# Own buffers for the first loads, the first weight's split on three engines, and the order of exponentials and copies on ScalarE

## What is computed

```python
scores = scale * q @ k.T
bias = -(cum[:, None] - cum[None, :])          # cum = cumsum(max(s, 0))
scores = where(causal, -1e9, scores + minimum(bias, 0))
attn = exp(scores - max); attn = attn / (sum + 1e-9)
x = attn @ v                                   # heads side by side: 2304 x 512
# first network (512 -> 1024 -> 512)
h = x @ w_in; solu = h * softmax(h); ln = (solu - mean) / sqrt(var + 1e-6) * g_ln
x2 = ln @ w_out
# second network (512 -> 2048 -> 512)
h = x2 @ w2_in; out = (h * clip(h + 3, 0, 6) / 6) @ w2_out
```

## Time and profile before

| what | value |
|---|---|
| median of 3 runs | 928.36 us (926.16 to 928.52) |
| profiled execution | 927.4 us, span 925.6 us |
| TensorE busy | 846.5 us (91%) |
| VectorE, ScalarE, GpSimd busy | 437.2, 407.7, 307.9 us |
| attention with the first network | up to about 449 us for the attention items |
| first hidden matmul | at 64.98 us |

### The profile page before, as it was taken

The page is one execution under the profiler, slowest core; times in us unless marked ns, Lnnn a source line. Parts: engine busy times, 40 slices in busy tenths (PEclk is TensorE's granted clock), DMA queues, the critical chain, the costliest instruction groups (busy, mean ns, idle before and its releaser), DMA issues.

```text
span 925.6 us, 13793 instructions
## 1 busy us (share of the span) xinstructions
PE 846.5 (91%) x4912; PEld 753.1 (81%) x4912; DVE 437.2 (47%) x1057; ACT 407.7 (44%) x901; POOL 307.9 (33%) x419
## 2 busy tenths in 40 slices
PE   5676878999899998999898999999999999999997
PEld 4555767878788887788787899999989898989996
DVE  3536677666676767766645232222232322232222
ACT  5636576656755566566323244322232322232222
POOL 5894375545654456545156244000000000000000
PEclk9879879999999999999999999999999999999999
DMA  6736333434333234322212040000000000000000
GB/s 180 222 101 206 99 104 120 136 94 116 119 119 95 85 117 131 108 93 72 72 65 93 1 137 1 35 1 1 34 1 1 35 1 1 35 1 1 35 1 34
DMA packets 39139, 67.11 MB, mean 73 GB/s; under 512 B 4448, under 2 KB 16736, under 8 KB 39072
## 3 DMA queue, kind: packets, MB, share of 16 engines
q1 hardware_dynamic: 39072, 66.23, 23.1%
HBM read 61.42 MB, written 4.79 MB: 72 GB/s over the span
## 4 chain that ended last, share of the span: by engine, by line
PE 71%; DVE 9%; ACT 8%; POOL 6%; issue 5%; DMA 1%; SPq 0%; DVEq 0%; ACTq 0%; POOLq 0%
PE psum L742 10%; PE psum L791 7%; PE psum L793 7%; PE psum L809 7%; PE psum L792 7%; PE psum L810 7%; PE psum L808 7%; PE psum L712 4%; PE psum L687 3%; PE psum L771 3%; DVE es L953 2%; PE psum L673 2%; ACT prob L1065 2%; ACT p_hi L1088 2%; PE psum L668 2%
## 5 line engine op out<-in xcount | busy, mean ns | idle before, releaser
L1019 DVE SCALAR_TENSOR_TENSOR act<-act,psum 128x384 f32<-128x384 f32 x96 | 53.2, 554 | 287.2 <-ACT act L1160 287.2
L1160 ACT ACTIVATE act<-psum,three 128x384 f32<-128x384 f32 x96 | 55.7, 580 | 285.8 <-PE psum L793 285.8
L791 PE MATMUL psum<-x_hi,w_hi 128*128 128x384 f32 x384 | 129.5, 337 | 0.9 <-DVE x_lo L979 0.9
L793 PE MATMUL psum<-x_hi,w_lo 128*128 128x384 f32 x384 | 129.5, 337 | 0.0
L792 PE MATMUL psum<-x_lo,w_hi 128*128 128x384 f32 x384 | 129.0, 336 | 0.0
L810 PE MATMUL psum<-w_hi,g_lo 128*128 128x512 f32 x288 | 113.9, 395 | 0.0
L809 PE MATMUL psum<-w_lo,g_hi 128*128 128x512 f32 x288 | 113.7, 395 | 0.0
L893 DVE TENSOR_TENSOR p_lo<-psum,p_hi 128x512 fp32r<-128x512 f32 (+2 forms) x128 | 71.9, 572 | 86.9 <-ACT p_hi L1088 86.4
L808 PE MATMUL psum<-w_hi,g_hi 128*128 128x512 f32 x288 | 112.0, 389 | 0.0
L1088 ACT ACTIVATE p_hi<-psum 128x512 fp32r<-128x512 f32 (+2 forms) x128 | 62.2, 499 | 111.3 <-PE psum L687 79.8
L771 PE MATMUL psum<-lnT_hi,w_out_hi 128*128 128x256 f32 x288 | 83.3, 289 | 12.4 <-DVE xT L975 12.4
(11 more groups left out here) (91 smaller groups left out, 1891.1 us busy)
## 6 DMA issues: line engine op xcount, KB each, us to landing
qk_raw<-qk SPq DMA_DIRECT2D x32, 480.0 KB, 3.5
qk_raw<-qk SPq DMA_DIRECT2D x32, 256.0 KB, 2.7
bias<-cum_dram SPq DMA_DIRECT2D x32, 256.0 KB, 3.9
v_raw<-v_rows SPq DMA_DIRECT2D x32, 160.0 KB, 2.7
bias_tail<-cum_dram SPq DMA_DIRECT2D x32, 144.0 KB, 3.2
out<-out_sb SPq DMA_DIRECT2D x6, 768.0 KB, 3.5
bias<-cum_dram SPq DMA_DIRECT2D x32, 128.0 KB, 3.4
w_raw<-w_in SPq DMA_DIRECT2D x16, 256.0 KB, 3.2
```

Source lines behind the costliest of these rows:

```text
L791: pe.matmul(ps, w2_hi[f][:, cols], xh, start=(c_ == 0), stop=False)
L793: last = pe.matmul(ps, w2_lo[f][:, cols], xh, start=False, stop=(c_ == NC - 1))
```

## The change

There are five parts. The eight loads of the first batch's first-kind units get buffers of their own, in the region that `w_out` takes later, so that they and the next three are issued without a wait, and the splits of queries and keys are placed one item earlier in general. The bias of the first unit comes from two TensorE matmuls (a column of the identity, broadcast, times `cum`) and two ScalarE copies in place of DMAs. `w_in` is loaded and split in 8 pieces: ScalarE makes all high parts, VectorE the first 4 low parts, GpSimd the other 4, and each hidden matmul of the first tile waits for its own piece. In ScalarE's loop the exponentials of item n+1 stand in front of `copy_probs(n)`. And `STARTS` moves tiles 0 to 9 up to two items earlier and ends one item earlier.

```diff
-STARTS = [14, 23] + [32 + 7 * i for i in range(4)] + [60 + 6 * i for i in range(8)] + [109, 116, 122, 128, 134]
+STARTS = [12, 21, 31, 37, 44, 51, 59, 65, 71, 77, 84, 90, 96, 102, 109, 115, 121, 127, 133]
...
-W_IN_PARTS = 16
+
+W_IN_PARTS = 8
+W_IN_DVE = 4
...
+OWN = HEADS
...
+def buffer_of(load):
+
+    return 3 + load if load < OWN else (load - OWN) % 3
...
-    SPLIT_AT.setdefault(BASE[_u] - (3 if _u % (2 * PAIRS) <= PAIRS else 4), []).append((_u, 0))
-    SPLIT_AT.setdefault(BASE[_u] - 2, []).append((_u, 1))
+    for _e in range(2):
+        if load_of(_u, _e) < OWN:
+            _n = max(-3, load_of(_u, _e) - 5)
+        elif _u == PAIRS:
+            _n = BASE[_u] - 5 + _e
+        elif _e == 1:
+            _n = BASE[_u] - 3
+        else:
+            _n = BASE[_u] - (4 if _u % (2 * PAIRS) <= PAIRS else 5)
+        SPLIT_AT.setdefault(_n, []).append((_u, _e))
...
+            def split_w_in(i):
+                pool.wait_ge(w_in_hi_done, i + 1)
+                pool.tensor_tensor(w_in_part(w_in_lo, i), w_in_part(w_in_raw, i), w_in_part(w_in_hi, i).bitcast(F32),
+                                   ALU.subtract).then_inc(w_in_lo_pool, 1)
+                return w_in_lo_pool, i - W_IN_DVE + 1
...
+                    if t == 0 and term == 0:
+                        if n // 3 < W_IN_DVE:
+                            pe.wait_ge(w_in_lo_dve, n // 3 + 1)
+                        else:
+                            pe.wait_ge(w_in_lo_pool, n // 3 - W_IN_DVE + 1)
...
+            pe.wait_ge(cum_done, 1)
+            for e in range(2):
+                pe.matmul(bank(H_BANK + e, CUT), ident[0:NH, e:e + 1].broadcast_to([NH, P]), cum[:, 0:CUT],
+                          start=True, stop=True).then_inc(bias_spread, 1)
...
+            def split_w_in(i):
+                dve.wait_ge(w_in_hi_done, i + 1)
+                dve.tensor_tensor(w_in_part(w_in_lo, i), w_in_part(w_in_raw, i), w_in_part(w_in_hi, i).bitcast(F32),
+                                  ALU.subtract).then_inc(w_in_lo_dve, 1)
...
+            def copy_bias(e):
+                sc.wait_ge(bias_spread, e + 1)
+                sc.activation(bias[e][:, 0:CUT], bank(H_BANK + e, CUT), ACT.Copy).then_inc(bias_copied, 1)
+
+            def split_w_in(i):
+                sc.wait_ge(w_in_loaded[i], 16)
+                sc.activation(w_in_part(w_in_hi, i), w_in_part(w_in_raw, i), ACT.Copy).then_inc(w_in_hi_done, 1)
...
-                if 0 <= n < ITEMS:
-                    copy_probs(n)
                 if 0 <= n + 1 < ITEMS:
                     for i, (tile, e, col) in enumerate(TILES[n + 1]):
                         exp_row(n + 1, i, tile, col)
+                if 0 <= n < ITEMS:
+                    copy_probs(n)
```

More of the change, by code:

```diff
@@ L208, in build, with qk_buffer @@
         qk_hi, qk_raw, qk_lo = [], [], []
+        def qk_buffer(stack, p, width):
+            qk_hi.append(sb(stack, f"qk_hi{p}", [P, width], F32R))
+            with nc.sbuf_tensor(f"qk_raw{p}", [P, width], F32) as raw:
+                qk_raw.append(raw)
+            qk_lo.append(sb(stack, f"qk_lo{p}", [P, width], F32R))
         for p in range(3):
[L210 to L213, removed]
+            qk_buffer(a_region, p, ST)
         v_sp = [sb(a_region, f"v_sp{p}", [P, NQ, 2, DH], F32R) for p in range(2)]
@@ L230, in build @@
         w_in_lo = sb(first, "w_in_lo", [P, NC, F1], F32R)
+        with ExitStack() as own:
+            for p in range(3, 3 + OWN):
+                qk_buffer(own, p, QW[1] + KN[1])
         w_out_hi = sb(first, "w_out_hi", [P, NF1, DM], F32R)
@@ L337, in build @@
         cum_stored = sem("cum_stored")
-        qk_loaded = [sem(f"qk_loaded{p}") for p in range(3)]
+        qk_loaded = [sem(f"qk_loaded{p}") for p in range(3 + OWN)]
         v_loaded = [[sem(f"v_loaded{p}{i}") for i in range(2)] for p in range(2)]
@@ L342, in build @@
         bias_tail_loaded = sem("bias_tail_loaded")
-        w_in_loaded = [sem(f"w_in_loaded{p}") for p in range(NC)]
+        w_in_loaded = [sem(f"w_in_loaded{p}") for p in range(W_IN_PARTS)]
         w_out_loaded = sem("w_out_loaded")
@@ L418, in head_of, with w_in_part, bias_loads @@
             return HEADS * b + 2 * p + e
+        def w_in_part(tensor, i):
+            half, c_ = i // NC, i % NC
+            return tensor[:, c_, half * BANK:(half + 1) * BANK]
+        def bias_loads(u):
+            return len(units_of_half(u)) - (1 if half_of(u) == half_of(0) else 0)
         def tokens(u):
@@ L471, in _ @@
             load_qk(0, 1)
+            load_qk(1, 0)
             sp.wait_ge(cum_done, 1)
             sp.dma_start(cum_dram, cum[:, :]).then_inc(cum_stored, 16)
-            load_qk(1, 0)
+            load_qk(1, 1)
             sp.wait_ge(cum_stored, 16)
[L476 to L481, removed]
+            for e in range(2):
+                load_bias(1, e)
+            load_qk(2, 0)
+            for e in range(2):
+                load_v(0, e)
+            load_qk(2, 1)
+            load_qk(3, 0)
+            for e in range(2):
+                load_v(1, e)
+            load_qk(3, 1)
             first_tail = min(u for u in range(UNITS) if not FIRST_KIND[u])
-            load_bias_tail(first_tail)
+            load_qk(first_tail, 0)
             for n in range(-2, BASE[UNITS] + 4):
-                for load in range(3, 2 * UNITS):
+                for load in range(OWN + 3, 2 * UNITS):
                     u_, e_ = (load - 3) // 2, (load - 3) % 2
@@ L616, in _ @@
             behind = consts_done, 4
-            w_in_next = 0
-            for n in range(-3, END + 1):
+            for n in range(-2, END + 1):
                 t, r = STEP_AT.get(n, (None, None))
-                if n in SPLIT_X_AT:
-                    behind = split_x(SPLIT_X_AT[n])
+                for u, e in SPLIT_AT.get(n - 1, ()):
+                    behind = split_qk(u, e, behind)
                 for u in range(UNITS):
@@ L626, in _ @@
                     behind = split_v(u, e)
+                if n in SPLIT_X_AT:
+                    behind = split_x(SPLIT_X_AT[n])
                 if r == 5:
                     behind = variance(t)
-                for u, e in SPLIT_AT.get(n, ()):
-                    behind = split_qk(u, e, behind)
-                for _ in range(1 if n < 8 else 2):
-                    if n >= W_IN_FROM and w_in_next < W_IN_PARTS:
-                        behind = split_w_in(w_in_next)
-                        w_in_next += 1
+                i = n - W_IN_FROM - 1
+                if W_IN_DVE <= i < W_IN_PARTS:
+                    behind = split_w_in(i)
                 if n >= EARLY_FROM and n - EARLY_FROM < 2 * EARLY:
```

56 lines of the change are left out of this document (34 added, 22 removed).

## The result

The changed kernel takes 958.5 us (median of 4 runs, 954.87 to 959.41), the one before 928.4: a ratio of 1.0322, 95% interval 1.0295 to 1.0348. It is slower, as forecast, but by 30 us and not by 8.5, and the time lies above the range of 911 to 952. The profiled execution has a span of 956.6 us against 925.6.

A forecast was written before the change was run, and what follows sets the result against it. GpSimd holds the front, short dependences among three engines beside a nine-tenths-busy TensorE the rest. Span 925.6 - 6.5 (front) + 13 (loop) + 2 (clock) = 934.1, so 936.9 us; range 911 to 952, forecast's own 931 to 952.

The forecast's parts named there:

- Exp(n+1), copy(n), split(n), row maximum n+2, exp(n+2) follow one another: Items 28 to end of attention: the loop has one item's time instead of two; 346 us for 333.2, a loss of 13.
- Rivals 1, 2 and 3: 1: loop hidden, 910, chance 0.14; 2: only step-4 items pay, 923, 0.14; 3: loop at lower bound, 926 to 931, 0.08.
- With idle time there up from 28.6 to 41 I add 2 us: Items 28 to end of attention: more TensorE idle time lowers the granted clock, costing 2 us.
- Rival 4: Middle of the kernel: clock falls often, 0.90 over 346 us, 12 us more, above 950; chance 0.08.
- The sum of the loop: Items 28 to 111: VectorE 216.8, exponentials 70.1, copies 46.6, hand-offs 2.5, together 336.0; with 10.4 for tile exponentials and squares, 346.
- above 1.3 us: Sign of being right, items 28 to 111: TensorE's waits average above 1.3 us, ended by exponentials and the projection copy.
- -6.5: Front, up to item 28: first-pair bias -1.8, items 12 to 15 -7, items 15 to 28 +2.3, a net gain of 6.5 us.
- near 8.0: Start of program: the first row maximum starts near 8.0 instead of 9.92, when item 0's scores end; gain 1.8 us.
- at most 0.1: Start of program: bias matmuls hidden in TensorE's free 1.67 us; at twice 0.45 us each they delay item 0 by 0.1.
- with the weight wait, GpSimd's lateness and the half-rate matmuls gone: Front, items 12 to 15: 11.5 us instead of 18.55, a gain of 7 us.
- Own buffers, earlier splits: Removes most of the 6.5 us TensorE waits before score matmuls; saving within the loop's loss, not counted again; late loads priced at nothing.
- Steps up to two items earlier: Nothing.: Table of first slots: from tile 10 on steps stand on the same items, the removed item held no work; worth nothing.

The follow-up runs named there:

- added VectorE work: An unused 384-column reduction ahead of each row maximum from slot 12 on: added to the changed kernel 986.4 us, to it with copy ahead of exponentials 927.3 us.
- copy first: Changed kernel with ScalarE's copy of item n's transposes again ahead of the exponentials of item n+1: 919.0 us, ratio to before 0.9911.
- order alone: Kernel before with only ScalarE's two blocks exchanged, exponentials of item n+1 ahead of the copy of item n's transposes: 960.1 us, ratio 1.0356.
- maximum ahead of the split: Changed kernel with VectorE taking the row maximum of item n+2 before the split of item n: 1052.7 us, ratio to before 1.1359.

## Why the prediction was right and where it failed

**In all.** Of the 31.0 us by which the span grew, the forecast had 8.5. Of the 22.5 that are missing, 14.0 lie in the long stretch, 7.1 in the front and 1.4 behind item 111.

**The order.** Right in kind. "Exp(n+1), copy(n), split(n), row maximum n+2, exp(n+2) follow one another" is what the timeline shows, ScalarE's idle time moved to where it was said to go, and the exchange alone makes the kernel slower. Rivals 1, 2 and 3 (910, 923 and 926 to 931) fall with it.

**Its size in the long stretch.** Mis-sized: the forecast was 346 us and 2 for the clock, in place of 333.2, so 15 lost, and it was 362.2, 29 lost. Of the 14 that are missing, some 5 are idle time (41 forecast, 46.1 found) and 9.5 are busy time. The term that failed most is the one on the clock: "With idle time there up from 28.6 to 41 I add 2 us" became 11.5 us of longer matmuls, of which 9.7 are the clock. Rival 4 ("The clock falls often in the middle", 12 us more, chance 0.08) had this size but took it to need 0.90; at 0.95 it was there. It counted only a third of the time lost at half rate as on the path; and by its own terms it gives 948.9 (936.9 + 12), not "above 950".

**The sum of the loop** was an average over items, and took one loop to bind everywhere, with light items making up for heavy ones. Less the 11.5 us of longer matmuls, the stretch took 350.7 us, so the sum of 346 came within 5 us. That is in part luck: added VectorE work was paid by half only, so the loop does not bind throughout, and the slots of steps 4 and 5 pay over twice as much as the rest. Where two bounds take turns, the mean of the larger one is above the mean of each.

**The link that was left out.** From item 13 on the transposes of an item wait for the split of the item before, since both use one PSUM bank (`before = n - 1` in `transpose_probs`). That is how the late copy reaches TensorE: 21.9 us in 20 waits, where the kernel before had in its own stretch of the earlier trace rows only

```profile
PE psum L687 <- DVE p_lo L893: 1.4, 2, 1.1
```

The prediction let the loop reach TensorE by the projection copy and the exponentials alone. In the long stretch of the changed kernel TensorE waited for exponentials not once, and its 42 waits lasted 1.1 us on average, where the prediction wanted exponentials among what ends them and "above 1.3 us".

**The front.** "-6.5" became +0.6 at item 28. Up to item 12, -0.15 in place of -1.8: the first row maximum and the first item came 1.3 us earlier (8.63, not "near 8.0"), since the bias matmuls took 2.04 us and pushed the scores by 0.55, more than "at most 0.1", and most of this was lost again by item 12, where the exchange costs 3.3 (50.33 against 47.03). From 12 to 15, -4.3 (18.55 to 14.26) in place of -7, and item 15 starts at 64.59, not near 60:

```profile
50.33:64.59 14.26, 12.26 (x62) 10.01 (x63) 5.19 (x15) 6.11 (x14) 7.50 (x8) 0.77 0.22 70
...
53.66 0.79 PE L794 MATMUL psum<-w_in_hi,xs_hi 128*128 128x512 f32 x1 [2.00 <-POOL xs_lo L655]
```

The step "with the weight wait, GpSimd's lateness and the half-rate matmuls gone" failed in its last two parts: the first hidden matmul still waits 2.00 us for GpSimd, now for the low part of the tile's input, two of GpSimd's weight pieces (from 45.84 and 48.38) still stand in the chain that ended last, and the granted clock is 0.77 (0.68 before, from 50.48 to 69.03), so half-rate matmuls are fewer but not gone. From 15 to 28 the loop cost 5.0 us (46.76 to 51.79) in place of 2.3; with the copy first it is 42.7. The loop's sum of 49.1 for it was 2.7 too low.

**"Own buffers, earlier splits": nothing beside the score waits.** Together they are worth 5.8 us once the copy stands first, about the 6.5 of the score waits, but not in the place of these: in the long stretch their removal gained 0.3 us, 2.5 came in the front, and the rest isn't located. The weight split is worth 4.8 us, though VectorE's and GpSimd's pieces ran at 1006 and 1314 ns.

**"Steps up to two items earlier: Nothing."** Wrong by 5 us, as measured with the copy first. The prediction looked at which engine has work in the slots and not at when the tile's input is ready: tiles 2 and 6 need the last unit of a batch, and now start in the very slot in which GpSimd splits their input.

**The sum again, from the runs.** Before 928.4; the three parts other than the order and the table give 913.9 (14.5 less, where the three undone one at a time make 11.6); the changed table +5.1, 919.0; the exchange +39.5, 958.5. The best version, copy first with before's table, is faster than both kernels.

**Open.** How much of the 11.5 us of longer matmuls lies on the path was not tried by itself; no kernel here changed the clock and nothing else. And which of several near-equal bounds holds each item was not shown.

## What to carry to other kernels

An idle stretch ahead of an instruction isn't free for the next piece in the queue: ScalarE idled 75.2 us before its copies, and it looked as if exponentials could be done there, but their own input, a row maximum, stands in VectorE's queue behind the split that the copy releases. With the exponentials in front, the wait moved and grew (86.6 us before exponentials), and 32 to 40 us were lost. Before pricing a moved step, list every wait of the engines behind it, bank reuse among them. When a step is started earlier, check where its slowest input is produced at the edges (the end of a batch), not in the steady state. And when an engine that is nine tenths busy is given more waits, count its clock too.

## What the runs showed of the chip

Longer matmuls are 11.5 of the 29 us lost in the long stretch, and 9.7 of them are the lower clock. In the changed kernel (windows of 4 us, columns as above) the stretch around the start of tile 2 reads:

```profile
124.00:128.00 4.00, 3.00 (x21) 2.48 (x19) 2.45 (x7) 3.29 (x10) 3.09 (x8) 0.87 0.31 103
128.00:132.00 4.00, 1.63 (x11) 1.31 (x11) 3.62 (x8) 1.41 (x3) 3.02 (x6) 0.98 0.54 142
132.00:136.00 4.00, 1.88 (x5) 1.49 (x5) 2.51 (x9) 3.34 (x9) 1.99 (x3) 0.50 0.00 0
136.00:140.00 4.00, 4.00 (x21) 3.41 (x20) 2.31 (x6) 0.53 (x4) 2.68 (x4) 0.67 0.04 4
```

From 128 to 132 us TensorE is busy 1.63 of 4 us, with a wait of 2.01 us that ends and one of 3.31 us that begins in it. In the next slice the granted clock is 0.50, which is 1.2 GHz, and it comes back to 2.4 GHz only within the slice behind that, in which TensorE is busy throughout. Over items 28 to 111 the same matmuls were busy 300.7 us at a mean clock of 0.97, 311.0 at 0.94, 312.9 at 0.95 and 345.7 at 0.90 (copy first, order alone, changed, maximum ahead of the split). By the clock records TensorE was busy at 1.2 GHz for 13.8, 35.0, 34.6 and 79.8 us of these. Half of the difference to copy first is what the lower clock cost: 10.6 us for order alone, whose matmuls were 10.3 us longer, but 10.4 in the changed kernel, where they were 12.2 longer, and 33.0 with the maximum ahead, where they were 45.0 longer and TensorE stood still over 0.1 us 103 times (38 with the copy first). What the rest is no run shows. The Trainium skill (TensorE: Matmul & The Clock Gate, Part 1) has activity lift the clock from a low default, and the trace agrees: the clock is 0.50 in the slice in which the second wait ends and rises in the slice in which TensorE is busy for 4.00 of 4 us.
